# Attention and two feed-forward layers: the first pair's queries and keys in halves, the weights split one step later

## The reference

```
scores = q @ k^T / 8, per batch and head (4 x 8), seq 576, head_dim 64
masked so that a block of 64 queries sees its own and earlier blocks
attn   = exp(scores - max) / (sum + 1e-9);  x = attn @ v        -> 2304 x 512
h = x @ w_in (512 x 2048);  g = softplus(h);  x = g @ w_out (2048 x 512)
skip/router: rows with x @ w_skip > 0 go to the best of 8 experts by x @ w_gate
out = x, or x + gate * (relu(x @ w1[e]) @ w2[e])
```

## Time and profile before

| what | us |
|---|---|
| median of 3 runs (lowest, highest) | 700.47 (699.14, 701.51) |
| the profiled execution, its own time | 700.94 |
| its span in the profile | 699.3 |
| attention (first load to the first hidden chunk) | 0 to about 195 |

### The profile page before, as it was taken

How to read it: one execution, slowest core, us unless ns; L and a number is a source line. 1 busy time by engine, 2 the same in 40 slices (tenths; PEclk the granted TensorE clock), 3 DMA queues, 4 the chain that set the end, 5 groups by cost and what they waited for, 6 DMA issues and landing times.

```text
span 699.3 us, 12929 instructions
## 1 busy us (share of the span) xinstructions
PE 676.8 (97%) x3990; PEld 521.2 (75%) x3990; DVE 433.3 (62%) x1049; ACT 404.5 (58%) x990; POOL 165.4 (24%) x227
## 2 busy tenths in 40 slices
PE   6999999999999999999999999999999999999895
PEld 4565555656578999889989998899888988864342
DVE  5566676767666676567656765676567656746122
ACT  3576666667775566656565656565656565542221
POOL 2767767676741000001000200020002000103111
PEclk9899999999999999999999999999999999999998
DMA  8355665554202000200020002000200010079170
GB/s 202 92 154 140 174 169 144 148 138 125 83 35 70 1 1 1 92 0 12 0 90 0 9 0 90 0 0 0 90 0 12 0 45 0 3 260 357 52 257 25
DMA packets 79439, 53.73 MB, mean 77 GB/s; under 512 B 61192, under 2 KB 64264, under 8 KB 79392
## 3 DMA queue, kind: packets, MB, share of 16 engines
q1 hardware_dynamic: 75952, 50.60, 24.1%
q0 software_dynamic: 1920, 1.73, 0.9%
q10 hardware_dynamic: 1520, 0.82, 0.4%
HBM read 41.18 MB, written 16.28 MB: 82 GB/s over the span
## 4 chain that ended last, share of the span: by engine, by line
PE 86%; DVE 4%; DMA 2%; issue 2%; SPq 2%; ACT 1%; POOL 1%; DVEq 0%; ACTq 0%; POOLq 0%
PE hidden L999 9%; PE hidden L1001 9%; PE hidden L1000 9%; PE rows_out L1012 9%; PE rows_out L1010 9%; PE rows_out L1011 9%; PE turned L352 8%; PE scores L333 6%; PE mixed L376 5%; PE scores L339 2%; PE hidden L1113 2%; PE rows_out L1128 2%; PE mixed L364 2%; DMA softplus_done<-x_sorted 1%; PE turned_y L1037 1%
## 5 line engine op out<-in xcount | busy, mean ns | idle before, releaser
L1221 ACT ACTIVATE mag<-hidden 128x384 f32<-128x384 f32 x96 | 47.3, 492 | 151.6 <-PE hidden L1001 149.8
L999 PE MATMUL hidden<-x_parts,w_in_high 128*128 (+1 forms) x384 | 132.8, 346 | 0.5 <-DVEq L1413 0.4
L1001 PE MATMUL hidden<-x_parts,w_in_low 128*128 (+1 forms) x384 | 129.4, 337 | 0.0
L1000 PE MATMUL hidden<-x_parts,w_in_high 128*128 (+1 forms) x384 | 129.4, 337 | 0.0
L948 POOL DMA_INDIRECT x_sorted<-y,slot x18 | 20.5, 1140 | 406.7 <-DVE slot L1462 403.1
L1012 PE MATMUL rows_out<-w_out_high,g_low 128*128 128x512 f32 x288 | 114.0, 396 | 0.0
L1010 PE MATMUL rows_out<-w_out_high,g_high 128*128 128x512 f32 x288 | 113.7, 395 | 0.4 <-DVE g_low L1420 0.4
L1011 PE MATMUL rows_out<-w_out_low,g_high 128*128 128x512 f32 x288 | 113.5, 394 | 0.0
L459 ACT ACTIVATE probs<-scores,neg_max 128x128 f32<-128x128 f32 (+3 forms) x128 | 67.1, 530 | 21.7 <-DVE neg_max L554 15.1
L269 POOL TENSOR_SCALAR probs<-probs,inverse 128x128 f32<-128x128 f32 (+3 forms) x128 | 66.9, 544 | 52.6 <-DVE inverse L575 52.6
L999 PEld LDWEIGHTS hidden<-x_parts,w_in_high 128*128 128x128 f32 x384 | 72.1, 188 | 8.3 <-issue 3.1
(11 more groups left out here) (179 smaller groups left out, 1058.0 us busy)
## 6 DMA issues: line engine op xcount, KB each, us to landing
whole_w<-in_moe_w_dram SPq DMA_DIRECT2D x12, 1024.0 KB, 11.3
x_heads<-x_pair SPq DMA_DIRECT2D x16, 288.0 KB, 2.1
x_raw<-x_heads SPq DMA_DIRECT2D x6, 768.0 KB, 5.6
out_dram<-y SPq DMA_DIRECT2D x6, 768.0 KB, 4.0
q_nat<-in_q_dram SPq DMA_DIRECT2D x32, 128.0 KB, 2.6
v_nat<-in_v_dram SPq DMA_DIRECT2D x32, 128.0 KB, 2.4
stage<-in_moe_w_in_dram SPq DMA_DIRECT2D x8, 512.0 KB, 3.9
stage<-in_moe_w_out_dram SPq DMA_DIRECT2D x8, 512.0 KB, 3.7
```

The lines of the kernel that those rows point to most:

```text
L999: nc.tensor.matmul(o, win["high"][:, k, cols], high, start=(k == 0), stop=False)
L1000: nc.tensor.matmul(o, win["high"][:, k, cols], low, start=False, stop=False)
L1001: last = nc.tensor.matmul(o, win["low"][:, k, cols], high, start=False, stop=(k == K - 1))
```

## The change

Six edits, numbered here as the prediction names them.

1. The first pair's q and k are loaded as chunks 0 and 1, then chunks 2 and 3 (64 KB a transfer, four on each queue); SyncE loads both ends after that. TensorE transposes the first halves into the two banks of `turned` and the second halves into the two banks of `mixed` (`turn_first`). VectorE copies q's halves, ScalarE k's. `score(0, 0)` and `score(0, 1)` wait for the first halves' copies only; `turn_qk(0, "ends")` comes behind them, its copy behind the first two maxima.
2. `WARM_FIRST` is 5, not 9.
3. `score(0, 3)` goes to `mixed` and waits for no exponents; `score(1, 0)` waits for pair 0's chunk 1 and not for its chunk 3.
4. `load_weights(1)` isn't issued ahead of the loop, and each later load comes one step later.
5. GpSimd splits piece p-1 in step p, between the two groups of scalings as before; in step 0 it splits none.
6. Piece 15 is loaded to the buffer `y` after attention and split by GpSimd after its constants; `rows_chunk` waits for it at f = 14 (five times, in blocks 0 to 4; block 5 has `last_rows`), and ScalarE's first copy of the rows of every block waits for it too.

```diff
-WARM_FIRST = 9
+WARM_FIRST = 5
+            if p == 0 and i == 3:
+                return mixed[:, :, 0:P * (i + 1)]
...
+            def load_first_q():
+                for half in range(2):
+                    c = slice(2 * half, 2 * half + 2)
+                    for two in range(2):
+                        sp.dma_start(q_nat[:, 0, c, two, :],
+                                     qf[two, 2 * half * P:(2 * half + 2) * P, :].rearrange("(c p) d -> p c d", p=P))\
+                          .then_inc(q_loaded[0] if half else s["first_half_loaded"], 16)
+                for nat, src in ((q_nat, qf), (k_nat, kf)):
+                    sp.dma_start(nat[0:TAIL, 0, FULL, :, :], src[0:2, FULL * P:S, :].rearrange("a p d -> p a d"))\
+                      .then_inc(ends_loaded[0], 16)
...
             load_weights(0)
-            load_weights(1)
...
-                if 0 < p < PAIRS - 1:
-                    load_weights(p + 1)
+                if 0 < p < LAST_PART:
+                    load_weights(p)
...
                     scale(FULL, 0)
+                    if p <= LAST_PART:
+                        split(p - 1)
                 if p < PAIRS:
-                    split(p)
...
-                if i == 0:
+                if p == 0 and i == 0:
+                    pe.wait_ge(s["copied_by_vector"], copies[-1, "q"][1])
+                    pe.wait_ge(s["copied_by_scalar"], copies[-1, "k"][1])
+                elif p == 0 and i == 2:
+                    pe.wait_ge(s["second_q_copied"], 1)
+                    pe.wait_ge(s["second_k_copied"], 1)
+                elif i == (0 if p > 0 else FULL):
                     pe.wait_ge(s["copied_by_vector"], copies[p - 1, "ends"][1])
-                if i != 1 and CH * p + i > 2:
-                    pe.wait_ge(s["probs_ready"], CH * p + (-1, None, 0, 2, 3)[i])
+                if i != 1 and CH * p + i > 2 and (p, i) != (0, 3):
+                    pe.wait_ge(s["probs_ready"], CH * p + (-1 if p > 1 else -3, None, 0, 2, 3)[i])
...
+            def turn_first(half):
+                if half == 0:
+                    pe.wait_ge(s["first_half_loaded"], 64)
+                else:
+                    pe.wait_ge(q_loaded[0], 32)
+                    pe.wait_ge(k_loaded[0], 32)
+                for n, nat in enumerate((q_nat, k_nat)):
+                    to = mixed[:, n, :] if half else bank(-1, "qk"[n])
+                    for c in range(2):
+                        last = nc.tensor.transpose(to[:, c * P:(c + 1) * P],
+                                                   nat[:, 0, 2 * half + c, :, :].rearrange("p a d -> p (a d)"), ident[:])
+                    last.then_inc(s["second_half_turned" if half else "turned_ready"], 1)
...
+            act.wait_ge(s["turned_ready"], turned_count(-1, "k"))
+            nc.scalar.copy(kT[:, 0, 0:2 * P], bank(-1, "k")[:, 0:2 * P]).then_inc(s["copied_by_scalar"], 1)
+            act.wait_ge(s["second_half_turned"], 2)
+            nc.scalar.copy(kT[:, 0, 2 * P:4 * P], mixed[:, 1, 0:2 * P]).then_inc(s["second_k_copied"], 1)
...
+            sp.wait_ge(att["mixed_right_ready"], PAIRS)
+            sp.dma_start(last_part.rearrange("p (f n) -> p f n", n=DM),
+                         w_out[LAST_F * P:(LAST_F + 2) * P, :].rearrange("(f p) n -> p f n", p=P))\
+              .then_inc(s["last_part_loaded"], 16)
...
+            pool.wait_ge(s["last_part_loaded"], 16)
+            high, low = (wout[h][:, LAST_F:F, :].rearrange("p f n -> p (f n)") for h in ("high", "low"))
+            nc.gpsimd.tensor_copy(high, last_part).then_inc(s["last_part_high"], 1)
+            pool.wait_ge(s["last_part_high"], 1)
+            nc.gpsimd.tensor_tensor(low, last_part, high, ALU.subtract).then_inc(s["last_part_split"], 1)
...
             def rows_chunk(n, f):
+                if f == LAST_F:
+                    pe.wait_ge(s["last_part_split"], 1)
...
                     act.wait_ge(x_stored, 16 * PAIRS)
+                    act.wait_ge(s["last_part_split"], 1)
```

More of the change, by code:

```diff
@@ L171, in attention @@
                 if step < PAIRS - 1 if name in ("q", "k", "ends") else step > 0:
-                    by = "copied_by_scalar" if name in BY_SCALAR else "copied_by_vector"
+                    by = "copied_by_scalar" if name in BY_SCALAR or (step, name) == (-1, "k") else "copied_by_vector"
                     units[step, name] = len(units)
@@ L196, in load_qk @@
                     sp.wait_ge(s["turned_ready"], turned_count(p - 3, "ends"))
-                for nat, src, loaded in ((q_nat, qf, q_loaded), (k_nat, kf, k_loaded)) if p > 0 else ((q_nat, qf, q_loaded),):
+                for nat, src, loaded in ((q_nat, qf, q_loaded), (k_nat, kf, k_loaded)):
                     for two in range(2):
@@ L231, in store @@
                   .then_inc(x_stored, 16)
-            load_qk(0)
+            load_first_q()
             load_qk(1)
@@ L384, in tensor @@
                 nc.tensor.matmul(scores[:, 0, 0:P], ident[:], ident[:], start=True, stop=True)
-            for name in ("q", "k", "ends"):
-                turn_qk(0, name)
+            for half in range(2):
+                turn_first(half)
             for p in range(PAIRS):
@@ L390, in tensor @@
                 score(p, 1)
+                if p == 0:
+                    turn_qk(0, "ends")
                 if turn:
@@ L436, in scalar @@
         def scalar(act, split_x):
[L438 to L441, removed]
-                .then_inc(ends_loaded[0], 16)
+            for half in range(2):
+                c = slice(2 * half, 2 * half + 2)
+                for two in range(2):
+                    nc.scalar.dma_start(k_nat[:, 0, c, two, :],
+                                        kf[two, 2 * half * P:(2 * half + 2) * P, :].rearrange("(c p) d -> p c d", p=P))\
+                        .then_inc(k_loaded[0] if half else s["first_half_loaded"], 16)
             nc.scalar.preload_act_table_set("natural_log_exp_and_others")
+            act.wait_ge(s["turned_ready"], turned_count(-1, "k"))
+            nc.scalar.copy(kT[:, 0, 0:2 * P], bank(-1, "k")[:, 0:2 * P]).then_inc(s["copied_by_scalar"], 1)
+            act.wait_ge(s["second_half_turned"], 2)
+            nc.scalar.copy(kT[:, 0, 2 * P:4 * P], mixed[:, 1, 0:2 * P]).then_inc(s["second_k_copied"], 1)
             def exponent(p, i, two):
@@ L601, in copy_qk @@
                 ins.then_inc(s["copied_by_vector"], 1)
-            for name in ("q", "k", "ends"):
-                copy_qk(0, name)
+            dve.wait_ge(s["turned_ready"], turned_count(-1, "q"))
+            nc.vector.tensor_scalar(qT[:, 0, 0:2 * P], bank(-1, "q")[:, 0:2 * P], SCALE, None, ALU.mult)\
+                .then_inc(s["copied_by_vector"], 1)
+            dve.wait_ge(s["second_half_turned"], 1)
+            nc.vector.tensor_scalar(qT[:, 0, 2 * P:4 * P], mixed[:, 0, 0:2 * P], SCALE, None, ALU.mult)\
+                .then_inc(s["second_q_copied"], 1)
             for p in range(PAIRS):
@@ L607, in vector @@
                 two_maxima(p)
+                if p == 0:
+                    copy_qk(0, "ends")
                 if turn:
@@ L642, in attention, with rest @@
     return sync, gpsimd, tensor, scalar, vector, s, turned_count
-def rest(nc, x_heads, x_sorted, out, w1, w2, ident, win, wout, x_raw, router,
+def rest(nc, x_heads, x_sorted, out, w_out, w1, w2, ident, win, wout, x_raw, router,
          x_stored, PAIRS, attended, feed, sem, sb, ps, sizes):
```

16 lines of the change are left out of this document (10 added, 6 removed).

## The result

The changed kernel takes 695.44 us (median of 5 runs, 694.6 to 696.1), before it 700.47 (5 runs, 699.14 to 701.77). The ratio is 0.9919, with a 95% interval of 0.9898 to 0.9939: 5.0 us less, where 6.3 were forecast (694.2, with a range of 692.5 to 697.8). The profiled execution took 695.93 with a span of 694.2, so 5.1 us less than the span of before. That profiled execution of before (700.94, mean granted clock 0.991) is not its typical one: of 63 further executions of the kernel before, timed beside the experiments, 42 lie at 698.7 to 700.3 with a mean clock of 0.994 to 0.998, and 21 at 700.6 to 702.8 with 0.989 to 0.996.

What follows compares the result with a forecast made beforehand. TensorE's own work (busy 97%) was taken to bound the kernel. Terms 1.7 + 0.9 + 2.1 + 1.8 - 0.2 = 6.3 us took the profiled 700.94 to 694.6; the median, 0.47 lower, gave 694.2 (range 692.5 to 697.8).

Steps and rivals of the forecast that it cites:

- Edits 1 and 2: At the start, half transfers and a shorter warm-up begin the first scores at 5.7, not 7.43: 1.7 us gained.
- The landing: First pair's second half loads land 2.7 us after an issue at about 2.5, so at 5.2 (bounds 4.9 to 5.9).
- Edit 3: In step 0, VectorE's 1.27 us wait for chunk 3's scores goes, less 0.4 for the ends' copies: net 0.9 us.
- Edits 4 and 5: In step 0, GpSimd scales right behind the inverses, with no weight split standing ahead: 2.1 us gained.
- The clock: In step 1, TensorE's clock stays full, recovering 1.8 of the 2.24 us that half clock cost.
- Edit 6: TensorE's five satisfied waits for the last weight piece, behind attention, cost 0.2 us in all (0 to 1).
- The clock falls anyway: Rival, chance 0.2: TensorE's clock still falls after the start, so the gain is 4.5 and the time 696.0 us.
- The halves come late: Rival, chance 0.1: second halves land at 5.9 and pair 1's loads catch TensorE; gain 3.4, time 697.1 us.
- Slower: Rival, chance 0.05: waits for the last weight piece stop TensorE's queue; at 2 us each, 704 us.
- eaten in step 1: Rival, chance 0.1: pair 2's later q load and step 1's work bind; gain under 2.1, about 699.5 us.

Runs made afterwards that it cites:

- seven products: The changed kernel with seven warm-up products (WARM_FIRST 7) instead of five; 695.05 us, ratio 0.9928.
- the second profile: The changed kernel timed and profiled again with no edit; 695.11 us, ratio 0.9925.
- experiments 5: The changed kernel with chunk 3's first scores back in the old banks, waiting for exponents as before; 696.45 us, ratio 0.9948.
- experiment 4: The changed kernel with whole q and k transfers, nine warm-up products and all first copies by VectorE; 696.80 us, ratio 0.9955.
- experiment 7: The kernel before with only the weight loads and splits moved later, including the last piece; 699.63 us, ratio 0.9992.
- Experiment 6: The changed kernel with nine warm-up products and weight loads and splits as before the change; 703.29 us, ratio 1.0044.
- experiment 8: Four variants of the changed kernel: inverses earlier, ScalarE copying pair 1's k, scores before second halves' transposes, the last two combined; 695.23, 696.33, 696.11, 695.26 us.
- k by ScalarE: The changed kernel with ScalarE, not VectorE, copying pair 1's turned k in step 0; 696.33 us, ratio 0.9940.

## Why the forecast was right, and where it was off

The sign, the place and most of the mechanism were right; one term was mis-sized. The terms below are differences between two profiled executions.

- **Edits 1 and 2, forecast 1.7, measured 0.09.** This is the step that failed. Of the 1.6 missing, 0.4 is the second halves' landing (transposes at 5.59, not 5.2). The rest is TensorE's half rate: from these transposes to the first scores it took 1.02 us, not 0.5, and the scores needed 1.76 to VectorE's mask, not 1.03. The prediction costed the four products by length alone and put nothing for the rate of the start. The slip is in its working: it takes ten of 18 warm-up rows to need 10/18 of 3.62 us, 2.0, but the first of those 18 rows are slow ones, and the ten took 2.50. In the one profile with seven products the same edit measured 1.35, but the six runs of that kernel have the changed kernel's median (695.05 and 695.11). So the half rate accounts for the missing time in the profile; that it cost the runs' median anything is not shown.
- **The landing.** The prediction took 2.7 us for the second halves, and 2.15 by the Trainium skill's sum for a transfer ("DMA: Bandwidth & Descriptors", "Anatomy of one DMA"). That section gives the sum for transfers which GpSimd issues; these were issued by SyncE and ScalarE. The first pair's eight half loads of the changed kernel landed 1.9 to 2.9 us after their issue, with medians of 2.3 (q) and 2.7 (k).
- **Edit 3, forecast 0.9, measured 0.82** in VectorE's chain of the profile (6.99 to 6.17 us from mask to the inverses' end), and 1.13 in the second profile (5.86). From mask to layer it is worth 1.7 to 1.9 (experiments 5, and 4 against 7), since it also frees pair 1's scores; in time 1.3 us with the halves (same chip) and some 2.6 without them (ratios 0.9955 and 0.9992).
- **Edits 4 and 5, forecast 2.1, measured 2.07** (17.62 - 15.45, less a hand-over of 0.1). Experiment 6 shows that nothing else pays without them, experiment 7 that they brought no time without the others.
- **The clock, forecast 1.8 of 2.24, measured 1.80** (10.89 to 9.09). That it agrees to the hundredth is chance: at the median the gain from the clock is likely smaller, since most executions of before have a higher mean clock (0.994 or more) than the one profiled (0.991). What is shown: in the profiles the clock stayed full there in all eleven with the split moved and fell in the three with the split ahead, and all eleven executions of the changed kernel have a mean clock of 0.996 to 0.998. In other kernels with the split moved it was lower in some executions (experiments 7 and 8).
- **Edit 6, forecast -0.2**: no cost seen; layer to end 503.67 and 504.2 in the two profiles of the changed kernel, 503.98 before.
- 0.09 + 0.82 + 2.07 + 1.80 = 4.78, which is the shift at pair 2 (4.78) and at the layer (4.79). It must be so, since each term is the shift that one stretch adds; the sum doesn't show that each edit alone is worth its term. The other 0.3 of the span is within what this stretch varies between profiles of the same kernel (503.67 and 504.23).
- **Luck.** The time came within 1.3 us of the forecast although 1.6 us of its terms were missing. The 0.2 us put down for edit 6 weren't spent, and 0.3 us of the span came from behind the layer, by nothing that was changed.
- **The rivals.** *The clock falls anyway*: not in the changed kernel. *The halves come late*: by 0.4, not 0.7, and no idle time of TensorE ends with one of pair 1's loads. "Slower" and "eaten in step 1" had nothing for them; pair 2's q caused no wait. In the runs' median the gain is 5.0 (4.7 when the kernel was timed again), close to the profile's.

## What to carry to other kernels

Of several waits in a row, removing one can bring nothing, or a loss, until the others are gone. Here the halves and the banks made the kernel slower by 3 us as long as the weight split stood behind them, and moving the split alone brought no time; split and banks together brought 2.7 to 3.1 us (experiment 4), and the halves 1.3 to 2.1 more. Count what an added transfer pushes back in its queue. When you shorten a warm-up, read the rate from the durations of equal rows and not from the clock column, and take more than one profile: the moment of the rise differs from run to run. And compare the profiled execution's time and clock with those of the other runs before you count terms from it.

## What the runs showed of the hardware

- At the start TensorE is at 1.2 GHz while the column PEclk shows 1.00, in all 14 profiles; rows of 128 columns take 421 ns, later 272. With the same nine products ahead, full rate came near 4.5 us in the profile of before and after 7.7 in that of experiment 7 (the ends' transposes of q still took 0.34 there, 0.24 before). The Trainium skill ("TensorE: Matmul & The Clock Gate", "Part 1: The HAM clock gate") says that cold is the default and that the moment of the rise varies; the traces agree with both. The prediction had used the page for the fall alone.
- A stretch of low clock 58 us before the end appears in two of 14 profiles (mean 0.57 over 4 us in k by ScalarE) and goes with 1.8 to 2.8 us more from layer to end. TensorE had stood idle for 1.80 and 1.89 us just before it. One profile has the same wait of 1.89 us and no fall, and in ten others the wait is 0.96 to 1.13 us, without a fall. At 18 us in the profile of before the clock fell at the end of an idle time of 1.71 us. Such falls can be part of the spread of the kernels here, which is larger than most of the single edits.
- ScalarE's and VectorE's copies of 256 columns from PSUM take 0.37 and 0.42 us, those of 512 columns 0.58 and 0.68 (k by ScalarE in step 0 of experiment 8, and VectorE's in the earlier trace rows).
